# A fused attention and mixture kernel: the first batch's attention in a new order, with wide denominators for two of its four pairs of heads

## The reference

```python
def phi(x):                      # attention, per head
    proj = x @ w_phi             # 64 -> 128 features
    proj = proj - max(abs(proj), axis=-1)
    return concatenate([exp(proj), exp(-proj)])
q_p, k_p = phi(q), phi(k)
num = q_p @ (k_p.T @ v)
den = q_p @ sum(k_p over tokens) + 1e-06
x = num / den                    # heads side by side: 576 x 512

xk, xr = mu * x + (1 - mu) * x_prev      # for mu_k and mu_r
k = relu(xk @ w_k)                       # 512 -> 1024
y = sigmoid(xr @ w_r) * (k * k @ w_v)    # 1024 -> 512

h = relu(y @ w_in)                       # 512 -> 1024
out = (h * sigmoid(conv3(h))) @ w_out    # convolution over tokens
```

## Time and profile before

| | |
|---|---|
| median of 3 runs | 1322.52 us (1322.43 to 1322.78) |
| profiled execution | 1324.45 us, its span 1322.7 |
| TensorE busy | 1291.4 us, 98% of the span |
| VectorE busy | 776.7 us, 59% |
| ScalarE busy | 551.1 us, 42% |
| DMA engines, hardware queue | 19.5% of the span |
| granted clock of TensorE, mean | 0.992 |

### The profile page before, as it was taken

One profiled execution on the slowest core, in us unless ns is written; L12 is line 12 of the kernel. 1 busy time (PEld: TensorE's weight loads), 2 busy tenths in 40 slices (PEclk: granted clock), 3 DMA queues, 4 the chain that ended last, 5 costly groups with the idle time before them and its releaser, 6 DMA issues.

```text
span 1322.7 us, 23315 instructions
## 1 busy us (share of the span) xinstructions
PE 1291.4 (98%) x9528; PEld 1147.3 (87%) x9528; DVE 776.7 (59%) x1342; ACT 551.1 (42%) x1015; POOL 2.4 (0%) x15
## 2 busy tenths in 40 slices
PE   7959999999999999999999999999999999999998
PEld 6749898889889899889988898999898898898897
DVE  6765465655746556646565575456583673763853
ACT  3525335344353352533534435444352443443442
POOL 0000000000000000000000000000000000000000
PEclk9979999999999999999999999999999999999999
DMA  4511211212221212121121221412102012012001
GB/s 148 167 48 49 77 43 54 76 43 61 64 63 57 61 55 67 49 76 42 55 76 45 61 63 34 128 51 86 44 24 76 6 64 76 1 68 76 0 33 40
DMA packets 92666, 79.63 MB, mean 60 GB/s; under 512 B 62736, under 2 KB 71056, under 8 KB 91536
## 3 DMA queue, kind: packets, MB, share of 16 engines
q1 hardware_dynamic: 92560, 78.14, 19.5%
HBM read 58.80 MB, written 19.02 MB: 59 GB/s over the span
## 4 chain that ended last, share of the span: by engine, by line
PE 84%; DVE 7%; ACT 5%; issue 3%; DMA 1%; SPq 0%; ACTq 0%; DVEq 0%
PE psm L498 39%; PE ps L498 23%; PE pso L1011 5%; PE pso L1010 5%; PE pso L1009 5%; PE psh L1009 3%; PE psh L1011 3%; PE psh L1010 2%; DVE conv L1132 2%; ACT h L1085 2%; ACT conv L1087 2%; DVE gated L1120 2%; DMA den<-den_scr 1%; DMA den_scr<-den_cols 0%; DVE mix L847 0%
## 5 line engine op out<-in xcount | busy, mean ns | idle before, releaser
L498 PE MATMUL psm<-xy_hi,wk_hi 128*128 128x288 f32 x512 | 156.0, 305 | 10.6 <-DVE xy_lo L866 5.3
L1009 PE MATMUL psh<-xy_hi,win_hi 128*128 128x288 f32 x512 | 152.4, 298 | 3.5 <-ACT h L1085 3.5
L498 PE MATMUL psm<-xy_lo,wk_hi 128*128 128x288 f32 x512 | 152.7, 298 | 0.0
L498 PE MATMUL psm<-xy_hi,wk_lo 128*128 128x288 f32 x512 | 152.3, 298 | 0.0
L498 PE MATMUL psm<-k_hi,wv_hi 128*128 128x288 f32 x512 | 151.8, 297 | 0.0
L1010 PE MATMUL psh<-xy_lo,win_hi 128*128 128x288 f32 x512 | 151.2, 295 | 0.0
L1011 PE MATMUL psh<-xy_hi,win_lo 128*128 128x288 f32 x512 | 151.2, 295 | 0.0
L498 PE MATMUL psm<-k_lo,wv_hi 128*128 128x288 f32 x512 | 151.0, 295 | 0.0
L498 PE MATMUL psm<-k_hi,wv_lo 128*128 128x288 f32 x512 | 150.8, 295 | 0.0
L871 DVE TENSOR_TENSOR k_lo<-square,k_hi 128x288 fp32r<-128x288 f32 x128 | 57.4, 454 | 135.0 <-ACT square L713 134.1
L1132 DVE SCALAR_TENSOR_TENSOR conv<-h,taps,conv 128x576 f32<-128x576 f32 x64 | 52.4, 818 | 141.9 <-ACT conv L1087 141.9
(11 more groups left out here) (129 smaller groups left out, 2716.8 us busy)
## 6 DMA issues: line engine op xcount, KB each, us to landing
qk<-in_k SPq DMA_DIRECT2D x32, 320.0 KB, 3.4
v_nat<-in_v SPq DMA_DIRECT2D x32, 320.0 KB, 3.5
qk<-in_q SPq DMA_DIRECT2D x32, 288.0 KB, 3.1
den<-den_scr SPq DMA_DIRECT2D x64, 144.0 KB, 3.0
y_scr<-y SPq DMA_DIRECT2D x64, 144.0 KB, 1.8
y<-y_scr SPq DMA_DIRECT2D x8, 1152.0 KB, 5.6
out<-rows SPq DMA_DIRECT2D x32, 256.0 KB, 2.0
stage<-in_moe_w_in SPq DMA_DIRECT2D x4, 512.0 KB, 4.2
```

Of the source, the lines that this page charges most:

```text
L498: return nc.tensor.matmul(o, lhsT, rhs, start=first, stop=last, skip_group_check=True)
L1009: nc.tensor.matmul(o, wh, xh, start=first, stop=False, skip_group_check=True)
```

## The change

The diff rewrites the first batch's attention.

- Queries and keys are projected in separate steps, F (`features_only`) and G (`keys_only`). F of pair p+1 stands between the two halves of pair p's sums (KV0 and KV1, `sum_kv` with one sign each), so that queries are projected a pair ahead of the keys.
- For pairs 2 and 3 (`WIDE = 2`) the denominators are computed over 64 repeated columns (`sum_den_wide`), so they stand in the same rows as the numerators; `copy_wide` copies both into tiles of their own. `divide_half` inverts and multiplies half of the tokens: D0 the first half, D1 the second. Spread, store and load by DMA are gone for these two pairs of the first batch; `sent` counts the semaphores anew.
- Pieces have three staging buffers, the third being `gate`, and steps of their own, SH on ScalarE and SL on VectorE.
- WARM is 7 matmuls before the first projection and 6 in pair 0; there are none in pairs 1 to 3.
- phi is loaded from ScalarE's queue; queries and keys of pair 1 are loaded at the start, and the pieces before mu. A small exponential loads ScalarE's table early. TensorE waits for `pick` at the first PICK instead of at the start.
- The next batch's first projection (NE) stands before DEN and NUM of pair 3. In the first iteration of the main loop D0 of pair 3 and the mixing of K for it come first, R's mixing and D1 of pair 2 beside M of pair 0, D1 of pair 3 beside PICK, and XK(1,0) beside QT of pair 1.
- Some waits are added in all batches: `turn_maxima` for the keys' tail, `shift_keys` for the last sums, `part_maxima` for the projected queries.

```diff
-WARM_FIRST, WARM = 24, 12
+WIDE = 2
+WARM_FIRST, WARM = 7, 6
...
+    steps = [("F", 0), ("G", 0), ("F", 1), ("EK", 0), ("QT", 0), ("WARM", 0), ("KV0", 0), ("M", 0)] + hi()
+    steps += [("EL", 0), ("QT", 1), ("KV1", 0), ("PICK", 0)] + hi()
+    for p in range(1, PAIRS):
+        steps += [("G", p), ("M", p), ("EK", p)] + ([("DV", p - 2)] if p >= 2 else []) + [("DEN", p - 1), ("NUM", p - 1)] + lo()
+        if p - 1 >= WIDE:
+            steps += [("D0", p - 1)]
+        steps += [("EL", p)] + hi() + [("KV0", p)]
+        if p + 1 < PAIRS:
+            steps += [("F", p + 1)] + lo() + [("QT", p + 1)] + [("RC", p - 1)] + [("KV1", p)] + lo() + [("PICK", p)] + hi() + hi()
+        else:
+            steps += lo() + hi() + [("KV1", p)] + lo() + lo() + [("PICK", p)]
+    return steps + mixing("K", 2, 0) + [("NE", 0), ("DEN", PAIRS - 1), ("NUM", PAIRS - 1)]
...
+BESIDE_SECOND = {
+    **BESIDE_NEXT,
+    ("M", 0): mixing("R", 0, 0) + mixing("R", 0, 1) + [("D1", WIDE)],
+    ("PICK", 0): [("D1", WIDE + 1)],
+    ("QT", 1): [("XK", 1, 0), ("RC", 0)],
+}
...
+            if step == ("E", 0) and batch == 0:
+                out += [("D0", PAIRS - 1)] + mixing("K", 0, 1)
...
+            if n >= 3:
+                sp.wait_ge(piece_lo, n - 2)
...
+                if kind == "SL" and step[1] + 3 < len(PIECES):
+                    load_piece(step[1] + 3)
...
         def turn_maxima(p, a):
             await_(pe, q_part_ready, PAIRS, a, p + 1)
+            await_(pe, k_tail_shifted, PAIRS, a, p + 1)
...
+        def sum_den_wide(p, a):
+
+            await_(pe, kvz_copied, PAIRS, a, p + 1)
+            await_(pe, q_exp_ready, 4 * PAIRS, a, 4 * p + 4)
+            for chunk in CHUNKS[1]:
+                cols = slice(*chunk)
+                for e in range(2):
+                    for h in range(2):
+                        mm(q_cols(1, p, a)[D * h:D * h + D, cols], kvz[:, e, h, D:D + 1].to_broadcast([P, D]), q_exp[:, e, h, cols], e == 0, e == 1)
...
+        def copy_wide(p, a):
+            await_(act, attended, PAIRS, a, p + 1)
+            nc.scalar.activation(den_first[:, p - WIDE, :], q_cols(1, p, a), ACT.Copy, bias=1e-6).then_inc(first_den, 1)
+            nc.scalar.activation(num_first[:, p - WIDE, :], q_cols(0, p, a), ACT.Copy).then_inc(num_copied, 1)
...
+        def divide_half(n, p):
+
+            cols, own = slice(HALF * n, HALF * n + HALF), p - WIDE
+            dve.wait_ge(first_den, own + 1)
+            nc.vector.reciprocal(den_first[:, own, cols], den_first[:, own, cols]).then_inc(first_inverse, 1)
+            dve.wait_ge(first_inverse, own + 1 + (PAIRS - WIDE) * n)
+            dve.wait_ge(num_copied, p + 1)
+            nc.vector.tensor_tensor(x[:, p, 1 + HALF * n:1 + HALF * n + HALF], num_first[:, own, cols], den_first[:, own, cols],
+                                    ALU.mult).then_inc(x_ready if n else x_half, 1)
```

More of the change, by code:

```diff
@@ L57, in first_attention_steps, with hi, lo @@
 def first_attention_steps():
[L59 to L69, removed]
+    rounded, lowered = itertools.count(), itertools.count()
+    def hi():
+        return [("SH", next(rounded))]
+    def lo():
+        return [("SL", next(lowered))]
+    steps = [("F", 0), ("G", 0), ("F", 1), ("EK", 0), ("QT", 0), ("WARM", 0), ("KV0", 0), ("M", 0)] + hi()
[10 more added lines that the diff above has]
+    return steps + mixing("K", 2, 0) + [("NE", 0), ("DEN", PAIRS - 1), ("NUM", PAIRS - 1)]
 def half_tiles(n):
@@ L104, in iteration @@
     tiles[0:3] = [("K-",) + t[1:] for t in tiles[0:3]] + [("K+",) + t[1:] for t in tiles[0:3]]
-    beside = BESIDE_NEXT if with_next else ALONE
+    with_next = batch < LAST
+    beside = ALONE if not with_next else BESIDE_NEXT if batch else BESIDE_SECOND
     out = []
@@ L464, in work @@
                                          allow_slow_non_contiguous=True).then_inc(both.taps_loaded, 16)
-                if kind == "NUM":
+                if kind == "NUM" and (m is not None or step[1] < WIDE):
                     spread_den(step[1], a)
@@ L547, in turn_maxima, with keys_only, keep_warm @@
+        def keys_only(p, a):
+            await_(pe, kvz_copied, PAIRS, a, p)
+            for t in range(TT - 1):
+                for h in range(2):
+                    last = key_tile(p, h, t)
+            last.then_inc(k_projected, 1)
+        def keep_warm(count):
+            for _ in range(count):
+                mm(ps1[:, 1, 0:P], ident[:], ident[:], True, True)
         def turn_maxima(p, a):
             await_(pe, q_part_ready, PAIRS, a, p + 1)
+            await_(pe, k_tail_shifted, PAIRS, a, p + 1)
@@ L641, in work @@
                 elif kind == "PICK":
+                    if step[1] == 0 and m is None:
+                        pe.wait_ge(pick_ready, 1)
                     subtract_maxima(step[1], a)
@@ L751, in work @@
                                          ACT.Copy).then_inc(both.piece_hi, 1)
[L752 to L754 removed]
+                elif kind == "SH":
+                    split_piece(step[1])
         batches(work)
@@ L919, in work @@
                     tile_v(step[1], step[2], m)
-                if m is None and kind in ("EK", "KV", "NUM") and pieces < len(PIECES):
-                    split_piece(pieces)
-                    pieces += 1
+                elif kind == "SL":
+                    split_piece(step[1])
         batches(work)
```

172 lines of the change are left out of this document (104 added, 68 removed).

## The result

The changed kernel takes 1305.46 us (median of 4 runs, 1303.6 to 1308.29); the kernel before, on the same chip, 1322.65. The ratio is 0.9869, with a 95% interval of 0.9857 to 0.9881. That is 17.2 us won, where 22.3 were forecast; the time lies in the range and in none of the rivals' bands but that of clock and DMAs (1304 to 1308). The profiled execution is the fastest of the four, 1303.6 us with a span of 1301.8, against 1322.7 before.

What follows compares the result with a forecast made beforehand. TensorE's own work bounds the main loop; gains lie in the first batch's attention. K(0,3) comes 24.5 us earlier, less 2.2 for clock: 22.3 off the 1322.7 span, and 1300.2 as median; range 1295.5 to 1308.

Steps and rivals of the forecast that it cites:

- clock and DMAs: Rival for the first batch: 14.05 us a pair instead of 12.6 and more cold stretches, 1304 to 1308 us; chance 0.20.
- The two waits: TensorE's waits of 5.3 and 4.3 us after the first 84 us; gains lie before and at them.
- a landing far after 57: Sign of being wrong: SyncE's queue lets a weight piece land far after 57 us; last piece's landing was forecast at 56.4.
- the offset of before: Step from profiled execution to median, taken from the kernel before: 1.95 us below, so 1302.1 gives 1300.2.
- the walk: First batch's pairs stepped through with priced engine work: K-(0,0) at 65.85, K(0,3) at 71.5, gain 24.5 us before clock.
- The clock charge: One cold stretch of TensorE on the path, before the next batch's projections: 2.2 us, gain from 24.5 to 22.3.
- The step that walked pair 2: Pair 2 of the first batch: TensorE idles 1.1 us at the maxima's turn, PICK at 43.05 us.
- The start: Before the first projection: wait for pick moved, queries start at 5.3 us, not 6.26, and reach VectorE at 7.3.
- The pieces: Piece 9 loads behind low part 6 (52.05), lands at 56.4; its high part delays kvz's copy and next projections to 57.9.
- Half divisions: VectorE's division for pairs 2 and 3: reciprocal over 288 columns 2.0 us, with the product 2.45 a half.
- The rival of a dear division: Above 2.8 us each reciprocal costs four times on the path: gain 5 to 16, 1306 to 1318 us; chance 0.10.
- Cover of the D1s: In the loop both D1 (4.9 us) delay square 6 and the numerator's copies, costing nothing, with 1.6 us to spare.

Runs made afterwards that it cites:

- after_again: The changed kernel run once more with no edit, on another chip beside the kernel before: 1307.95 us, 0.9881 of the kernel before.
- v_first: The changed kernel with the load of the next pair's values issued ahead of the denominators' store and load in the first batch: 1305.1 us.
- d1_double: The changed kernel with each of the two D1 reciprocals made twice: 1309.8 us.
- warm_fill: The changed kernel with ten, four and six identity matmuls put back where TensorE idles, before sums of pairs 2 and 3 and the next batch's projections: 1301.68 us.
- start_only: The kernel before with only the change's start (seven identity matmuls, phi's queue, early exponential table, later wait for pick): 1323.54 us, 0.9998 of the kernel before.
- r_early: The changed kernel with R's mixing of pairs 0 to 2 moved back ahead of the next batch's keys on VectorE: 1308.56 us.

## Why the prediction was right, and where its sizes were off

- **What bounds, and the mechanism: right.** The two waits are gone, K-(0,0) starts 13.6 us earlier and K(0,3) 19.3, and from 79 to 340 us TensorE waits for nothing. In the profiled executions the span fell by 20.9, more than the 19.3 because the tile that before started at 95.97 was cold there (0.53 over 95.9 to 99.4) and is not now.
- **The number: in the range, above the forecast's own band.** The median lies above 1297.5 to 1304, which had the chance 0.53, and in the band of the rival "clock and DMAs bite more" (0.20). The last piece landed at 61.4, where a landing far after 57 stood as a sign of being wrong.
- **The own time is partly luck.** K(0,3) was forecast at 73.7 (71.5 and the 2.2 of the clock) and came 2.9 us later. The sum had nothing for the cold stretch behind 95.97, which is gone: 1.6 us the other way.
- **The step from the profiled execution to the median failed.** I took the offset of before, 1.95 us under its profiled execution. The own time was forecast as 1302.1 and measured as 1303.6, 1.5 off; but this execution is the fastest of its set and the median lies 1.9 above it, where I had it 1.95 below: that is 3.8 of the 5.3 us by which the median was missed, and 1.5 the walk. Beside it and beside after_again the kernel before ran at 1322.1 to 1325.0 with a mean clock of about 0.992; the changed one spreads over 1303.6 to 1309.7, and its mean clock over 0.999 to 0.993. Its fastest execution was not a typical one: the other three have a mean clock of 0.995 to 0.997 against its 0.999. So this point and the next are largely the same thing seen twice.
- **The clock charge was mis-sized.** Charged: one stretch, 2.2 us, at the next batch's projections. There was none there in the first trace (1.46 us idle before them), one behind the wait for the values (3.4 us at 1.2 GHz), and some 13 us in after_again. Filling the idle places is worth 3.8 us against the first set and 6.3 against after_again, so the term was some 2 to 4 us too small. The rival "clock and DMAs bite more" had this. My reason against it was that VectorE hides part; in the first trace it hid nothing there, since VectorE itself waits 3.29 us for TensorE (45.92).
- **A moved queue position was missed.** The step that walked pair 2 had values loaded in time; their load stands behind the denominators' store and loads, 2.55 us of idle time and 0.96 for pair 3. v_first removed the wait; in the median that is 2.9 us against after_again and 0.4 against the first set.
- **The start.** Queries started at 5.25 (5.3 forecast), but the tail's maximum ran at 8.78, not 7.4: TensorE stayed at half rate longer. The gain of the start by itself, 2 us at the first PICK, was worth nothing in the kernel before, and I have no run of the change without it.
- **The pieces: mechanism right.** Piece 9 was issued directly behind low part 6 (57.40; forecast 52.05) and its high part stands before the copy of kvz. It is 5.3 us late because x of pair 1 and low part 6 are, and those because of the stretch before; from the last PICK to K- the walk was 0.35 too long.
- **Half divisions: right.** 1.94 us for 288 columns, 2.0 forecast. The rate of about 6 ns a column beside a fixed 0.16 stands. The Trainium skill's repeat count of 8 (VectorE: DVE Perf Modes, "First, the fixed hardware budget") had given an estimate of 2.4 us; the measurement decides for 1.94. The rival of a dear division is out.
- **Cover of the D1s: right, but thin.** Forecast 1.6 us, in the trace 1.0: the numerator is copied at 93.45 and TensorE wants its bank at 94.42. d1_double adds 1.94 twice, 3.9, and shows 2.5 us, so a cover of 1.4.
- **The table load: right, 1.28 us** at 1.96, in idle time. The exponential follows the shift of the keys directly.
- **Wide denominators: 4.12 us with the numerator** instead of 3.9, twice: 0.4 in all.
- **Which part carries the gain: open.** Undone one at a time, the third buffer, the projection ahead and the wide denominators cost 11.6, 10.5 and 12.0 us against 1305.46 (9.2, 8.0 and 9.6 against 1307.95). They don't add up to the 17.2 of the change: each undoing opens idle time, and the clock falls behind it (0.78 to 0.84 over 12 to 95 us). How much of each is wait and how much clock isn't settled; for that each would need a run with fillers.

## What to carry to other kernels

Walk every in-order queue through the new order, not only the engines: a load that stood early can end up behind a store that must wait for something, here for 4 us. When idle places of one to three microseconds replace filler work on TensorE, price the cold stretches as a spread and not as one event, and put fillers into exactly these places before judging the order. A buffer's worth is not told by the last piece alone: walk every load that one buffer less moves back in the queue, and the engine that consumes it in order.

## What was unexpected in the hardware

- **The start can stay at half rate for a time that differs between executions of the same code.** The seven score matmuls of the first projection took 2.62 us in the change; in d1_double, whose instructions are the same up to there, they took 1.67:

```profile
6.32 1.67 PE L534 MATMUL ps<-qk,phi 64*128 64x512 f32 x7
```

  The first PICK came at 17.12 there, at 17.65 in the change, 19.28 in after_again and 22.18 in warm_fill. The granted clock reads 1.00 over the first 15 us of the change and the first 18 of warm_fill, so the durations, not PEclk, tell it. Why it differs is open.
- **Short idle stretches had half clock behind them, but not always:** 2.55 us of it in the change (40.11), 2.57 in start_only (49.35) and 1.66 in v_first (43.25) had; 2.82 in r_early (40.74) and the 1.46 before the next batch's projections in the change had none. So the length of the idle stretch alone doesn't tell. My charge had counted on one such place and there were others.
- **A reciprocal costs by its columns:** 1.94 us for 288 against 0.22 for 9, where a tensor_tensor of 288 columns takes 0.46.
